# A shorter cosine chain, two heads' scores side by side, and an MLP output with columns on partitions

## The chip, the cores and the metric

The kernel runs on one core of a Trainium2 chip, in one launch. TensorE (PE) multiplies matrices and writes PSUM, VectorE (DVE), ScalarE (ACT) and GpSimd (POOL) work on SBUF and, but for GpSimd here, on PSUM, and SyncE (SP) issues the DMAs. The metric is the device time of the launch in microseconds. All engines run programs of their own in a fixed order and wait for each other by counters (semaphores).

## The reference

Attention over 4 batches, 8 heads, 576 positions and 64 columns, then two MLPs over 2304 tokens of 512 columns:

```python
def _attn_ref(q, k, v):
    factor = 4
    # mean over groups of 4 positions, full softmax attention on 144, repeated 4 times
    out_d = sm_attn(q_d, k_d, v_d)
    out_up = np.repeat(out_d, factor, axis=2)
    # plus attention in a band
    mask = np.abs(pos[:, None] - pos[None, :]) < factor
    scores = np.where(mask, scale * np.matmul(q, k.transpose(0, 1, 3, 2)), -1000000000.0)
    ...
    return out_up + out_local

def _moe_ref(x, w_in, w_out):          # d_ff 2048
    h = x @ w_in
    return (h * np.cos(h)) @ w_out

def _moe2_ref(x, w_gate, w_val, w_out, rms_g):   # d_ff 1536
    xn = x / np.sqrt(np.mean(x * x, axis=-1, keepdims=True) + 1e-06) * rms_g
    g = xn @ w_gate
    return (g / (1 + np.exp(-g)) * (xn @ w_val)) @ w_out
```

## The kernel before

**Stages.** Batch 0's attention comes first, with buffers of its own for every pair of heads (`Wide`). Then the first MLP runs over six chunks of 384 tokens; during chunks 0 to 2 the attention of batches 1 to 3 (`Narrow`, one set of buffers) is threaded between its steps. The second MLP runs over three chunks of 768 tokens, 12 units each, 36 iterations `i`, with the seven products of Strassen-Winograd type for gate and value (`product`) and the output tiles of the iteration before as fillers (`down2`). Each f32 operand of a large matmul is split into a high and a low part in `F32R`, and three matmuls (`three`) give one product.

**First MLP.** A unit `f` of 16 has a first layer, `up` (4 x 3 matmuls of 384 columns into a bank `HB`), and a second, `down`, three steps later. Before, `down` has the hidden values as stationary operand and writes three banks `YB` with tokens on partitions, nine matmuls of 512 columns. Between them, `cosines` (ScalarE) and `hidden` (VectorE) make g = h cos h: ScalarE adds a magic constant to h / 2 pi (L751), VectorE takes turns off (L1053, L1055), ScalarE takes the absolute value and the sine (L757, L759), VectorE multiplies (L1061), ScalarE writes the high part (L686) and VectorE the low (L972). The first layer of unit f may write its bank once the product of unit f-3 has read it (`g_done`).

**Attention in a chunk.** A pair of heads goes through steps placed by hand at (unit, half): TensorE's scores of head 0 (`local` for the band in ten windows, `downsampled` for the 144 means), then of head 1, `transposes` of each head's probabilities, `values`. They share banks X and Z, so head 1's scores wait for head 0's to be read. VectorE subtracts maxima, sums up and adds both attentions into XY (L893), ScalarE takes exponentials (L617, L626), GpSimd sums values of four positions (`value_sums`, L495 and L500) and normalises (L507, L510).

**After a chunk.** `squares` on ScalarE sums y's squares by token, GpSimd makes the reciprocal root (L549) and scales y (`scale_y`, L553). Because y has tokens on partitions and the second MLP needs columns there, TensorE turns the scaled y (`turn`, four transposes each, L1348): six turns in chunk 5, twelve in the second MLP, and VectorE copies them out with the gain (`turn_out`, L1006). From these come seven operands, each split in two parts (`operand_high`, `operand_low`).

**Weights of the second MLP.** During chunks 3 to 5 ScalarE, GpSimd and DMAs split 84 weight operands (`weight_high`, L722; `gate_sum`; `weight_low`, L578), two a unit, through three buffers `wp`, and store them.

Of the kernel before, what the change touches and what calls it, by code (L numbers as in the profile page):

```python
# [7 lines left out]
BF16 = mybir.dt.bfloat16  # L8
ACT = mybir.ActivationFunctionType
# [5 lines left out]
P = 128  # L15
# [4 lines left out]
DM = H * D  # L20
# [23 lines left out]
NWP = NP * F2  # L44
QT = SD // 2
# [36 lines left out]
def attention_and_two_mlps(nc, qk, vwin, vgrp, w1, wgv, w2, rms_g, const, wsplit, out):  # L82
# [41 lines left out]
    ssq = keep("ssq", [P, TT], F32)  # L124
    msq = keep("msq", [P, TT], F32)
    rinv = keep("rinv", [P, TT], F32)
    mhalf = keep("mhalf", [P, TT], F32)
    ones = keep("ones", [P, 1], F32)
    spare = keep("spare", [P, 4], F32)
# [27 lines left out]
    xa = at("xa", [P, KT, CH], F32, slots_at)  # L157
    xb = at("xb", [P, KT, CH], F32, slots_at + KT * CH * 4)
    xt = at("xt", [P, 3, 2, CH], F32, slots_at + 2 * KT * CH * 4)
    xo = at("xo", [P, NP, 2, 2, CH], F32R, slots_at + 5 * 4096 + 1024)  # L160
# [3 lines left out]
    wp = [at(f"wp{i}", [P, 2, 256], F32R, a) for i, a in enumerate((prep_at + 11264, prep_at + 13312, yn_at))]  # L164
# [15 lines left out]
    X, Z = ps[:, 3, :], ps[:, 7, :]  # L180

    NH = 3
    HB = [ps[:, i, 0:CH] for i in range(NH)]
    YB = [ps[:, 4 + i, :] for i in range(TT)]

    CA, CB = ps[:, 1, 0:CH], ps[:, 2, 0:CH]
    Y2 = [ps[:, i, :] for i in (3, 7, 0, 4, 5, 6)]

    def turn_bank(c, t):
        return ps[:, 2, :] if c else ps[:, (3, 7)[t % 2], :]  # L190
# [14 lines left out]
    class Narrow:  # L205
# [4 lines left out]
        sl, sd = [X[:, 0:TP * WIN]] * 2, [Z[0:QT, 0:2 * SD]] * 2  # L210
# [39 lines left out]
    turns_ready = sem("turns_ready")  # L250
    angle0 = sem("angle0")
    angle_ready = sem("angle_ready")
    abs_ready = sem("abs_ready")
# [6 lines left out]
    ssq_ready = sem("ssq_ready")  # L260
    ms_ready = sem("ms_ready")
    rinv_ready = sem("rinv_ready")
    y_scaled = sem("y_scaled")
    tr_done = sem("tr_done")
    turned = sem("turned")
# [9 lines left out]
    wp_stored = [sem(f"wp_stored{i}") for i in range(3)]  # L275
# [41 lines left out]
    def y_tile(c, t):  # L317
        return XY[:, bass.ds(c * (TT * 512) + t * 512, 512)]
# [4 lines left out]
    XSRC = [xa[:, 0:2, :], xa[:, 2:4, :], xt[:, 1], xt[:, 0], xb[:, 0:2, :], xt[:, 2], xb[:, 2:4, :]]  # L323
# [7 lines left out]
    POOL_XO = (1, 3, 5)  # L331
    XO_ORDER = ((0, 1, 3, 2, 4, 5, 6), (0, 1, 2, 3, 4, 5, 6))
    DVE_OUT, ACT_OUT = (0, 2, 4), (1, 3, 5)
    TURN_F = 1
    TURN_STEP = 5
# [26 lines left out]
    def steps_at(names, where, place):  # L362
        return [(name, j) for j in range(PAIRS) for name, at_ in zip(names, where[j]) if at_ == place]
# [6 lines left out]
    def sync_program(sp):  # L370
# [86 lines left out]
        for i in range(3):  # L457
            hold(sp, wp_stored[i], 16 * NWP // 3)
# [1050 lines left out]
```

## Time and profile before

| what | value |
|---|---|
| median of 3 runs | 992.53 us (990.57 to 994.08) |
| profiled execution, its own time | 996.6 us |
| its span in the trace | 994.5 us |
| TensorE busy | 960.3 us (97%) |
| VectorE, ScalarE, GpSimd busy | 575.5, 502.1, 313.2 us |
| mean granted clock of TensorE | 0.99 |

The span is the stretch from the first to the last instruction of one execution; its own time has the launch around it. Busy is the time in which an engine has an instruction in flight; matmuls overlap, so their durations add up to more than that, and the distance of their starts is their price. Most matmuls on f32 data appear as two records each. PEclk is the clock granted to TensorE as a share of full speed.

### The profile page before, as it was taken

The numbers are of one execution on the slowest core, as the hardware profiler recorded it, in microseconds if no ns is written. First come the engines' busy times: TensorE is split into PE (matmuls) and PEld (weight loads), VectorE is DVE, ScalarE is ACT, GpSimd is POOL, SyncE is SP. The second block draws the span as 40 slices with busy tenths as digits, with TensorE's granted clock in tenths as the row PEclk, the third lists the DMA queues.
The fourth block names the chain that finished last, engine by engine and source line by source line (L and its number), as shares of the span: only waits on it lengthen the run. The fifth ranks groups of instructions, "written<-read, shape, count | busy, mean of one in ns | idle before, by whom it ended". The sixth has DMA issues, their size and how long they took to land.

```text
span 994.5 us, 17685 instructions
## 1 busy us (share of the span) xinstructions
PE 960.3 (97%) x6104; PEld 853.5 (86%) x6104; DVE 575.5 (58%) x1225; ACT 502.1 (50%) x1081; POOL 313.2 (31%) x366
## 2 busy tenths in 40 slices
PE   7889999999999999999999899999999999999998
PEld 6677787888888899899989789999899899999997
DVE  6767677676666665555656644445744445544434
ACT  4456566666666667676765433334522224433322
POOL 5947773221322147467575121111300001000000
PEclk9999999999999999999999899999999999999999
DMA  9522111211111025445344575555565555575531
GB/s 306 192 94 93 55 52 36 70 52 53 52 53 53 23 100 177 149 159 180 132 166 149 190 258 153 151 150 162 151 215 150 150 166 160 156 226 158 161 106 64
DMA packets 66174, 132.31 MB, mean 133 GB/s; under 512 B 7088, under 2 KB 7216, under 8 KB 66096
## 3 DMA queue, kind: packets, MB, share of 16 engines
q1 hardware_dynamic: 66096, 131.27, 42.0%
q8 instruction: 50, 0.82, 0.3%
q14 instruction: 28, 0.23, 0.1%
HBM read 104.50 MB, written 26.74 MB: 132 GB/s over the span
## 4 chain that ended last, share of the span: by engine, by line
PE 78%; DVE 8%; ACT 6%; issue 4%; POOL 4%; DMA 1%; DVEq 0%; ACTq 0%; POOLq 0%; SPq 0%
PE ps L1274 24%; PE ps L1276 24%; PE ps L1275 24%; DVE ub L1053 2%; POOL W L521 2%; PE ps L1193 2%; DVE ub L1055 1%; ACT ub L757 1%; PE ps L1210 1%; ACT ub L759 1%; PE ps L1348 1%; DVE XY L893 1%; PE ps L1227 1%; ACT probd L626 1%; DVE ub L1061 1%
## 5 line engine op out<-in xcount | busy, mean ns | idle before, releaser
L1274 PE MATMUL ps<-xo,wu 128*128 128x384 f32 x504 | 169.7, 337 | 5.2 <-ACT gate_a L806 3.7
L1275 PE MATMUL ps<-xo,wu 128*128 128x384 f32 x504 | 170.7, 339 | 0.0
L1276 PE MATMUL ps<-xo,wu 128*128 128x384 f32 x504 | 170.1, 338 | 0.0
L1274 PE MATMUL ps<-xs,W 128*128 128x384 f32 x384 | 134.6, 350 | 1.4 <-DVE xs L968 1.4
L1276 PE MATMUL ps<-xs,W 128*128 128x384 f32 x384 | 130.8, 341 | 0.0
L1275 PE MATMUL ps<-xs,W 128*128 128x384 f32 x384 | 130.3, 339 | 0.0
L1274 PE MATMUL ps<-W,ring 128*128 128x512 f32 x288 | 118.0, 410 | 0.0
L1276 PE MATMUL ps<-W,ring 128*128 128x512 f32 x288 | 115.0, 399 | 0.0
L1275 PE MATMUL ps<-W,ring 128*128 128x512 f32 x288 | 114.8, 399 | 0.0
L1274 PEld LDWEIGHTS ps<-xo,wu 128*128 128x128 f32 x504 | 95.4, 189 | 12.4 <-ACT gate_a L806 4.1
L1275 PEld LDWEIGHTS ps<-xo,wu 128*128 128x128 f32 x504 | 95.2, 189 | 6.7
L1061 DVE TENSOR_TENSOR ub<-ub,ps 128x384 f32<-128x384 f32 x96 | 53.0, 552 | 74.0 <-ACT ub L759 74.0
L1276 PEld LDWEIGHTS ps<-xo,wu 128*128 128x128 f32 x504 | 95.3, 189 | 0.0
L757 ACT ACTIVATE ub<-ub 128x384 f32<-128x384 f32 x96 | 50.4, 525 | 72.5 <-DVE ub L1055 72.5
L1276 PE MATMUL ps<-wo,ring 128*128 128x512 f32 x216 | 85.7, 397 | 0.0
L1275 PE MATMUL ps<-wo,ring 128*128 128x512 f32 x216 | 85.4, 395 | 0.0
L1274 PE MATMUL ps<-wo,ring 128*128 128x512 f32 x216 | 85.2, 395 | 0.1
L1274 PEld LDWEIGHTS ps<-xs,W 128*128 128x128 f32 x384 | 73.2, 191 | 6.8 <-DVE xs L968 1.9
L1101 DVE TENSOR_TENSOR val_b<-val_b,ps 128x384 f32<-128x384 f32 x36 | 20.0, 554 | 101.1 <-ACT val_b L806 100.9
L1275 PEld LDWEIGHTS ps<-xs,W 128*128 128x128 f32 x384 | 73.3, 191 | 1.9
L1053 DVE TENSOR_SCALAR ub<-ub 128x384 f32<-128x384 f32 x96 | 47.3, 493 | 47.5 <-ACT ub L751 47.5
L1276 PEld LDWEIGHTS ps<-xs,W 128*128 128x128 f32 x384 | 73.1, 190 | 0.0
(134 smaller groups left out, 1853.3 us busy)
## 6 DMA issues: line engine op xcount, KB each, us to landing
wu<-wsplit SPq DMA_DIRECT2D x252, 256.0 KB, 2.8
wsplit<-wp SPq DMA_DIRECT2D x84, 256.0 KB, 2.0
W_raw<-w SPq DMA_DIRECT2D x8, 1024.0 KB, 14.1
qk<-qk SPq DMA_DIRECT2D x14, 576.0 KB, 4.1
gv<-wgv SPq DMA_DIRECT2D x12, 512.0 KB, 3.6
vw<-vwin SPq DMA_DIRECT2D x14, 384.0 KB, 3.2
out<-XY SPq DMA_DIRECT2D x18, 256.0 KB, 3.4
vg<-vgrp SPq DMA_DIRECT2D x26, 144.0 KB
```

Of the source, the lines that this page charges most:

```text
L521: g.tensor_tensor(lo, raw, hi.bitcast(F32), ALU.subtract).then_inc(unit_ready, 1)
L626: ins = a.activation(kind.probd[j][0:QT, s, t, :], kind.sd[s][:, t * SD:t * SD + SD], ACT.Exp, scale=SCALE_D, bias=dbias[0:QT, s, t:t + 1] ...
L757: a.activation(v, v, ACT.Abs).then_inc(abs_ready, 1)
L759: a.activation(v, v, ACT.Sin, scale=-1.0, bias=consts[:, 1:2]).then_inc(cos_ready, 1)
L893: ins = v.tensor_tensor(XY[:, bass.ds(first, m)].rearrange("p (n r) -> p n r", r=FACTOR), kind.pv[r][:, src:src + m].rearrange("p (n r) -> ...
L1053: v.tensor_scalar(w, w, MAGIC, -2.0 * math.pi, ALU.subtract, ALU.mult).then_inc(angle0, 1)
L1061: v.tensor_tensor(w, w, HB[f % NH], ALU.mult).then_inc(g_done, 1)
L1101: v.tensor_tensor(vb[:, :], vb[:, :], CB, ALU.add).then_inc(vb_ready, 1)
L1193: ins = t_.matmul(sl[64 * half:64 * half + 64, t * WIN:t * WIN + WIN], q[:, Q0[w]:Q0[w] + WIN], k[:, K0[w]:K0[w] + WIN], start=False, stop ...
L1274: t_.matmul(dst, a_lo, b_hi, start=first, stop=False, skip_group_check=True)
L1275: t_.matmul(dst, a_hi, b_lo, start=False, stop=False, skip_group_check=True)
L1276: return t_.matmul(dst, a_hi, b_hi, start=False, stop=last, skip_group_check=True)
```

## The change

1. The cosine: VectorE alone forms the turns from PSUM (h / 2 pi arrives scaled, since x is scaled where it is split), and ScalarE keeps the sine and the high part. `HB` has two banks, and the first layer of unit f waits for the product of unit f-2. The first layer of the next chunk's unit 0 moves ahead of this chunk's last second layer.
2. Scores of both heads stand side by side, head 0's in bank X, head 1's in bank Z, window by window. The steps of a pair are placed anew, with one pattern for all pairs.
3. `down` has the weights as stationary operand and writes y with columns on partitions into four banks, twelve matmuls of 384 columns. There are no turns.
4. Squares: GpSimd multiplies and adds up y's four parts, splits the sum (nine steps, `squares`), TensorE sums over partitions with a matrix of ones (`stats`), VectorE makes the reciprocal root from a bit trick and three Newton steps and scales y with the gain (`rms_step`).
5. Six `wp` buffers in place of three, nine operand slots in place of seven; operands of the second MLP's first chunk are made from step 5 of chunk 5 on, all low parts on VectorE.

```diff
-    NH = 3
+    NH = 2
     HB = [ps[:, i, 0:CH] for i in range(NH)]
-    YB = [ps[:, 4 + i, :] for i in range(TT)]
+    YB = [ps[:, 2 + k, 0:CH] for k in range(KT)]
+    STATS = X[:, 0:CH]
...
+        def squares(c, steps=range(2 * KT + 1)):
+            for n in steps:
+                k, adds = (n + 1) // 2, n and n % 2 == 0
...
+                elif adds:
+                    g.tensor_tensor(sq[:, 0, :], sq[:, 0, :], sq[:, 1, :], ALU.add).then_inc(sq_ready, 1)
...
+                    g.tensor_tensor(sq[:, min(k, 1), :], y_part(c, k), y_part(c, k), ALU.mult).then_inc(sq_ready, 1)
...
         batch(1, (5, 5, 5, 1))
         with pool.Fori(2, B) as b:
+            squares(b - 2)
             batch(b)
+        squares(ACH - 1)
...
+                for c, first in ((ACH, NP * 4), (ACH + 1, NP * 9)):
+                    if 0 <= NP * f + p - first <= 2 * KT:
+                        squares(c, (NP * f + p - first,))
...
-                a.activation(v, HB[f % NH], ACT.Identity, scale=INV_2PI, bias=consts[:, 0:1]).then_inc(turns_ready, 1)
...
-                a.activation(v, v, ACT.Abs).then_inc(abs_ready, 1)
-                act.wait_ge(abs_ready, F1 * c + f + 1)
-                a.activation(v, v, ACT.Sin, scale=-1.0, bias=consts[:, 1:2]).then_inc(cos_ready, 1)
+                a.activation(v, v, ACT.Sin, scale=-2.0 * math.pi, bias=consts[:, 1:2]).then_inc(cos_ready, 1)
...
-                v.tensor_scalar(w, w, MAGIC, -2.0 * math.pi, ALU.subtract, ALU.mult).then_inc(angle0, 1)
+                v.tensor_scalar(w, HB[f % NH], 0.25, MAGIC, ALU.add, ALU.add).then_inc(angle0, 1)
...
+                if before and not last and STAT + attention < f <= STAT + RMS_STEPS:
+                    rms_step(c - 1, f - STAT - 1)
...
-            return three(YB[t], ring[:, f % 3, 0, cols], ring[:, f % 3, 1, cols], w_part(slot, 0), w_part(slot, 1), f == 0, f == F1 - 1)
+            return three(YB[k], w_part(slot, 0)[:, cols], w_part(slot, 1)[:, cols], ring[:, f % 3, 0, :], ring[:, f % 3, 1, :], f == 0, f == F1 - 1)
...
+                if c and attention and step == 3:
+                    pe.wait_ge(exp_down, 2 * PAIRS * (c + 1) + 2)
+                    stats(c - 1, STATS)
+                elif c and not attention and not last and step == STAT:
+                    stats(c - 1, STATS)
```

The order of instructions shows three places. The first is TensorE in chunk 0, between the first layers of units 1 and 2, where the first pair's scores stand. Before (L1187 to L1190 are the masks, L1193 the ten windows of head 0, L1210 its downsampled scores):

```order
L1187 MATMUL ps<-maskb,identb 128x64 [waits qk_in,x_ready]
L1188 MATMUL ps<-maskb,identb 128x192
L1190 MATMUL ps<-maskb,identb 128x64
L1193 MATMUL ps<-qk_77 64x64 x10
L1210 MATMUL ps<-qkd_83 72x144 [waits qkd_ready]
L1210 MATMUL ps<-qkd_83 72x144
L1274 MATMUL ps<-xs,W_49 128x384 [waits g_done,unit_ready]
```

Now (L1192 to L1195 are the masks, L1201 the windows):

```order
L1192 MATMUL ps<-maskb,identb 128x64 [waits qk_in,x_ready]
L1193 MATMUL ps<-maskb,identb 128x192
L1195 MATMUL ps<-maskb,identb 128x64
L1192 MATMUL ps<-maskb,identb 128x64
L1193 MATMUL ps<-maskb,identb 128x192
L1195 MATMUL ps<-maskb,identb 128x64
L1201 MATMUL ps<-qk_80 64x64 x20
L1310 MATMUL ps<-xs,W_49 128x384 [waits g_done,unit_ready]
```

The windows of both heads come in one run, and the downsampled scores have moved behind the next first layer.

The second place is GpSimd's loop over batches 2 and 3, at the head of its body. Before, the loop begins at once with the value sums of the first pair:

```order
L557 UNCONDITIONAL_BRANCH
L557 ISA
L495 TENSOR_TENSOR vg_79<-vg_79 72x2x128 [waits vg_in]
L342 ISA
L500 TENSOR_TENSOR vd_80<-vg_79 72x2x64 [waits vt_ready,pv_done]
```

Now the last part of the squares (L567 adds a part, L561 and L564 split the sum) stands ahead of the value sums (L504, L509):

```order
L574 ISA [waits sq_ready,y_copied_act]
L574 TENSOR_TENSOR sq<-XY 128x384
L361 REGISTER_ALU
L567 TENSOR_TENSOR sq<-sq 128x384 [waits sq_ready]
L361 REGISTER_ALU
L561 TENSOR_TENSOR sums_of_sq<-sq,ones 128x384 [waits sq_ready,stat_done]
L361 REGISTER_ALU
L564 TENSOR_TENSOR sums_of_sq<-sq,sums_of_sq 128x384 [waits sshi_ready]
L361 ISA [waits sslo_ready]
L504 TENSOR_TENSOR vg_82<-vg_82 72x2x128 [waits vg_in]
L361 ISA
L509 TENSOR_TENSOR vd_83<-vg_82 72x2x64 [waits vt_ready,pv_done]
```

Nine steps of squares, of which these are the last four, have moved ahead of the first pair.

The third place is VectorE in chunks 1 and 2 at units 9 and 10, where the third pair's scores are handled. Now (L1068 and L1070 are the first two passes of the cosine, L883 the downsampling of q and k, L917 to L919 the downsampled maximum, L1009 to L1013 a Newton step):

```order
L883 TENSOR_REDUCE qkd_86<-qk_80 128x288 [waits down_scores,qk_in]
L1008 REGISTER_ALU
L1009 TENSOR_TENSOR sq<-rms 128x384 [waits newton]
L1010 REGISTER_ALU
L1011 TENSOR_TENSOR sq<-sq 128x384 [waits newton]
L1012 REGISTER_ALU
L1013 SCALAR_TENSOR_TENSOR rms<-sq,rms 128x384 [waits newton]
L1065 REGISTER_ALU
L1068 TENSOR_SCALAR ub<-ps 128x384 [waits glo_ready,up_done]
L1070 SCALAR_TENSOR_TENSOR ub<-ub,ps 128x384 [waits angle0]
L917 TENSOR_REDUCE dmax<-ps 72x2 [waits down_scores]
L919 TENSOR_SCALAR dbias<-dmax 72x2 [waits dmax_ready]
```

Before, the downsampling of the next pair stood at the previous pair's last step, ahead of the sums into XY (L893):

```order
L1055 TENSOR_TENSOR ub<-ub,ps 128x384 [waits angle0]
L943 COPY probd_82<-ps 72x288 [waits pt_done]
L880 REGISTER_ALU
L884 TENSOR_REDUCE qkd_83<-qk_77 128x288 [waits down_scores,qk_in]
L972 TENSOR_TENSOR ring<-ub,ring 128x384 [waits ghi_ready]
L1061 TENSOR_TENSOR ub<-ub,ps 128x384 [waits cos_ready]
L889 REGISTER_ALU
L893 ISA [waits od_ready]
L893 TENSOR_TENSOR XY<-ps,od_84 128x116
```

The downsampling has moved behind both heads' differences, and a Newton step of three passes follows it, ahead of the next unit's cosine.

## Rows read from the trace of the kernel before

**Rows 1.** The page's section 1: busy us, share of the span, instructions of each engine.

```profile
PE 960.3 (97%) x6104; PEld 853.5 (86%) x6104; DVE 575.5 (58%) x1225; ACT 502.1 (50%) x1081; POOL 313.2 (31%) x366
```

**Rows 2.** Windows of chunks 0, 1 and 4: length, busy of each engine, clock, DMA.

```profile
55.00:157.00 102.00, 97.19 (x797) 81.58 (x798) 71.83 (x182) 61.36 (x132) 61.95 (x65) 0.97 0.22 72
157.00:254.00 97.00, 94.10 (x803) 79.49 (x802) 66.29 (x176) 62.62 (x136) 25.68 (x37) 1.00 0.17 54
417.80:484.60 66.80, 66.80 (x337) 60.63 (x337) 38.18 (x71) 46.73 (x107) 45.48 (x56) 1.00 0.45 161
```

**Rows 3.** Timeline of TensorE in chunk 3: start, duration, line, tiles; first matmul of each layer.

```profile
401.26 0.39 PE L1274 MATMUL ps<-W,ring 128*128 128x512 f32 x1
...
403.34 0.33 PE L1274 MATMUL ps<-xs,W 128*128 128x384 f32 x1
...
405.45 0.39 PE L1274 MATMUL ps<-W,ring 128*128 128x512 f32 x1
```

**Rows 4.** The same in chunk 0: one head's scores, and the values of both.

```profile
61.73 0.20 PE L1187 MATMUL ps<-maskb,identb 128*128 128x64 bf16 x1
...
62.71 0.71 PE L1210 MATMUL ps<-qkd 64*72 64x144 f32 x4
...
63.35 0.44 PE L1274 MATMUL ps<-xs,W 128*128 128x384 f32 x1
...
80.27 0.71 PE L1243 MATMUL ps<-probd,vd 72*64 72x144 f32 x8
80.91 0.91 PE L1251 MATMUL ps<-prob,vw 64*64 64x58 f32 x40
81.75 0.50 PE L1274 MATMUL ps<-W,ring 128*128 128x512 f32 x1
```

**Rows 5.** Timeline: turns in chunk 5 and the second MLP, and L1096 without turns.

```profile
503.42 0.60 PE L1348 MATMUL ps<-ident,XY 128*128 128x128 f32 x4
503.78 0.42 PE L1274 MATMUL ps<-xs,W 128*128 128x384 f32 x1
...
583.27 0.63 PE L1348 MATMUL ps<-ident,XY 128*128 128x128 f32 x4
...
595.53 0.63 PE L1348 MATMUL ps<-ident,XY 128*128 128x128 f32 x4
...
861.46 0.55 DVE L1096 TENSOR_TENSOR gate_a<-gate_a,ps 128x384 f32<-128x384 f32 x1 [0.57 <-PE ps L1276]
...
872.97 0.56 DVE L1096 TENSOR_TENSOR gate_a<-gate_a,ps 128x384 f32<-128x384 f32 x1 [1.18 <-PE ps L1276]
```

**Rows 6.** Waits of TensorE: total, times, longest, us.

```profile
PE ps L1274 <- ACT gate_a L806: 3.7, 1, 3.7
...
PE ps L1187 <- DVE XY L893: 3.7, 5, 1.4
...
PE ps L1210 <- ACT probd L626: 3.6, 3, 1.7
...
PE ps L1348 <- DVE xa L1006: 2.2, 1, 2.2
```

**Rows 7.** Timeline of GpSimd at the start of chunk 1: value sums, normalising.

```profile
164.53 0.73 POOL L495 TENSOR_TENSOR vg<-vg 72x256 f32<-72x256 f32 x1
...
169.69 0.45 POOL L500 TENSOR_TENSOR vd<-vg 72x128 f32<-72x128 f32 x1 [0.18 <-POOL vg L495]
...
172.27 0.72 POOL L507 TENSOR_TENSOR prob<-prob,recip 128x320 f32<-128x320 f32 x1 [2.13 <-DVE recip L938]
173.18 0.67 POOL L510 TENSOR_TENSOR probd<-probd,recip 72x288 f32<-72x288 f32 x1 [0.18 <-POOL prob L507]
```

**Rows 8.** Groups by line and form: count | busy us, mean ns | idle before.

```profile
L578 POOL TENSOR_TENSOR wp<-gv,wp 128x256 fp32r<-128x256 f32 x48 | 38.9, 811 | 32.6 <-ACT wp L722 29.8
...
L884 DVE TENSOR_REDUCE qkd<-qk 128x288 f32<-128x1152 f32 x14 | 18.8, 1346 | 2.2 <-DMA qk<-qk 2.2
...
L1055 DVE TENSOR_TENSOR ub<-ub,ps 128x384 f32<-128x384 f32 x96 | 53.2, 554 | 3.3
```

More of the change, by code:

```diff
@@ L456, in sync_program @@
                 load_gv(f + 2)
-        for i in range(3):
-            hold(sp, wp_stored[i], 16 * NWP // 3)
+        for i in range(WPN):
+            hold(sp, wp_stored[i], 16 * NWP // WPN)
         for n in range(RING):
@@ L631, in exps @@
         def exps(kind, b, j, s):
-            if kind is Narrow and s == 0:
+            if kind is Narrow:
                 exp_of_down(kind, b, j, s)
@@ L688, in attend @@
         def attend(c, f, half):
-            for what, j in steps_at(BESIDE_STEPS, BESIDE_WHERE, (f, half)):
+            for what, j in steps_at(ACT_STEPS, ACT_AT, (f, half)):
                 if what == "exps":
@@ L1199, in downsampled, with downsampled_tile, scores @@
+        def downsampled_tile(kind, j, s, t):
+            q, k = (kind.qkd[j][64 * s:64 * s + 64, a, :] for a in range(2))
+            return t_.matmul(kind.sd[s][:, t * SD:t * SD + SD], q[:, t * QT:t * QT + QT], k, start=True, stop=True)
+        def scores(kind, b, j, s):
             n = PAIRS * b + j
             u = 2 * n + s
+            if u > 1:
+                pe.wait_ge(diff_ready, u - 1)
+            if s == 0:
+                pe.wait_ge(kind.qk_in[j], 16 * loads(kind, b, j))
+            masks(kind.sl[s])
+            for w in range(NW):
+                ins = local_window(kind, j, s, w)
+            ins.then_inc(local_scores, 1)
@@ L1201, in downsampled @@
             if s == 0:
                 pe.wait_ge(qkd_ready, n + 1)
[L1203 to L1206 removed]
+            if u > 1:
                 pe.wait_ge(exp_down, u - 1)
[L1208 removed]
             for t in range(2):
[L1210 removed]
+                ins = downsampled_tile(kind, j, s, t)
@@ L1211, in downsampled, with local_both @@
             ins.then_inc(down_scores, 1)
-        def scores(kind, b, j, s):
-            local(kind, b, j, s)
-            downsampled(kind, b, j, s)
+        def local_both(kind, b, j):
+            n = PAIRS * b + j
+            pe.wait_ge(x_ready, n)
+            pe.wait_ge(kind.qk_in[j], 16 * loads(kind, b, j))
+            for s in range(2):
+                masks(kind.sl[s])
+            for w in range(NW):
+                for s in range(2):
+                    ins = local_window(kind, j, s, w)
+            ins.then_inc(local_scores, 2)
@@ L1217, in transposes, with downsampled_both @@
+        def downsampled_both(kind, b, j):
+            n = PAIRS * b + j
+            pe.wait_ge(qkd_ready, n + 1)
+            pe.wait_ge(diff_ready, 2 * n + 2)
+            for t in range(2):
+                for s in range(2):
+                    ins = downsampled_tile(kind, j, s, t)
+            ins.then_inc(down_scores, 2)
         def transposes(kind, b, j, s):
             n = PAIRS * b + j
+            if kind is Narrow and j == 0 and s == 0 and b > 1:
+                pe.wait_ge(ms_ready, b - 1)
```

506 lines of the change are left out of this document (246 added, 260 removed), and 6 rows, old and new, of tables (BESIDE_WHERE, PE_WHERE).

## The prediction

> **What bounds it now.** I read the busy shares first: TensorE is busy for 960.3 of 994.5 us [rows 1]. The windows by chunk show where it isn't: 4.8 us idle in chunk 0 and 2.9 in chunk 1, which carry attention of the next batch, and none in chunk 4, which doesn't [rows 2]. VectorE is busy for 66 to 72 us of an attention chunk of about 100, ScalarE for 61 to 63, GpSimd for 62 in chunk 0 and 26 in chunk 1. So TensorE's own work sets the time, and a change gains what it takes off that stream and loses every wait that it puts in. The timeline gives the price of that work, the waits what is to be had: the table of waits holds single waits of 3.7 and 2.2 us around the second MLP's begin, 3.7 for attention's sums and 3.6 for the exponentials [rows 6].
>
> **The cosine chain.** It takes two of ScalarE's passes from each of 96 units and leaves VectorE three of them plus the low part, as before, 0.55 us each [rows 8]. In chunk 4 TensorE doesn't wait for this chain at all [rows 2], so the shorter chain itself is worth nothing. Its cover is the distance of two or three units between a unit's first layer and its second; with two PSUM banks for h in place of three, unit f+2 now waits for the product of unit f, which has a second layer and a first layer (4.2 us) to be made: three passes of 0.55, a sine and a low part of about the same are 2.8. If that cover went, each late unit would cost its lateness.
>
> **Columns on partitions in the first MLP's y.** Nine matmuls of 512 columns become twelve of 384. By [rows 3] nine take 403.34 - 401.26 = 2.08 us and twelve 405.45 - 403.34 = 2.11, so 96 units lose 0 to 3 us; I take 2.0.
>
> **No transposes.** The 18 turns go. The six in chunk 5 take 0.36 us each; the twelve in the second MLP make an iteration 12.26 instead of 11.51 us, 0.75 each [rows 5]: 2.2 + 9.0 = 11.2 us gained. Instead TensorE adds up squares: two matmuls of 384 columns for each of six chunks, 0.175 each [rows 3], 2.1 us, and 0.35 more for each of the two that wait for CB as the turns did: 2.8 us.
>
> **Both heads side by side.** One head's scores now take from 61.73 to 63.35, 1.62 us: 0.25 for the masks, 0.73 for ten windows, 0.64 for two downsampled tiles, and entries. Two heads take 3.3 per pair. The values step already alternates tiles of the array: 20 matmuls in 81.75 - 80.91 = 0.84 us, twice the rate of the windows, and four tiles of 144 columns in 80.91 - 80.27 = 0.64, twice the rate of the downsampled scores [rows 4]. If the new order reaches these rates a pair costs 0.5 + 0.84 + 0.64 = 2.0 to 2.1 and saves 1.24; 12 pairs save 14.9 us. The bounds are 0 and 14.9; I take the upper, since the new order alternates halves of both rows and columns. The Trainium skill (TensorE: Matmul & The Clock Gate, Part 3) has weights load beside a running matmul only when the row group differs, which would leave the old order without this overlap and give it to the new one; the trace agrees in the two rates, but shows no pair of row groups alone.
>
> **Waits taken away.** More room (six wp buffers, nine operand slots, operands scaled two chunks ahead) moves the second MLP's operands early, so I drop the 3.7 and the 2.2 us [rows 6]: 5.9 us gained. Of attention's 3.7 for the sums I drop 2.5: the addition no longer stands behind the downsampling of q and k.
>
> **Waits put in.** Here most of the gain goes.
> (a) GpSimd, start of chunks 1 and 2. Its program now does nine steps of 384 columns for the squares before anything of the next batch. 256 columns take 0.81 us [rows 8], so 384 take 0.81 to 1.22, I take 1.08 with the gap: 9.7 us, from 0.9 us after the last second layer (one product and one copy). Behind them the first pair's value sums take 170.14 - 164.53 = 5.6 us, a DMA in their middle, and the first head's normalising 1.6 [rows 7]: the first transposes can't start before 0.9 + 9.7 + 5.6 + 1.6 = 17.8 us. TensorE's own work up to there is three first layers (6.3), the scores (2.1), the sum (0.35) and one second layer (2.1): 10.9. It idles for 6.8 us in each of the two chunks, 13.6 us. Before, GpSimd had these sums done long before the first pair's transposes, and rescaled y in 3 x 1.1 us.
> (b) Chunk 0 has no squares. But reduction of q and k (1.35 us [rows 8]) now stands behind two heads' differences, a low part and a product, and the exponentials one step later; in the first two steps there is no second layer that hides it. TensorE waited 1.2 us a time there [rows 6]; with 1.35 more it waits some 2.3 for the downsampled scores and 2.1 for the transposes: 4.4 us. From (a) and (b), 18.0 us, the old 3.6 goes off.
> (c) In the last pair of each attention chunk both heads' transposes follow each other with no first layer between (unit 16 doesn't exist). The second needs both copies of the first, which stand behind a product: the product's 0.55 [rows 8], a copy that is no longer than that, and the hand-over, some 1.3 us, three times: 4.0.
> (d) VectorE's Newton steps, three dependent passes of 0.59 with the gap (1.8 us), stand behind steps 8, 9 and 10 of chunks 1 and 2, the middle pair's scores. VectorE has 97 - 66.3 = 31 us free per chunk [rows 2], but in these steps it is what the transposes wait for. Between 0 and 5.3 us per chunk; I take 3: 6.0.
> (e) Chunk 4: the squares are dealt out between the weights, one after each of nine. Nine weight steps and five gate sums at 0.82, and nine squares at 1.08, from 1.9 us after the chunk's begin: 1.9 + 11.5 + 9.7 = 23.1. TensorE asks for the sums at step 6, after six first layers and three second ones: 9 x 2.1 = 18.9. It waits 4.2 us (0 to 5).
> (f) The clock stood at half in part of chunk 0 (0.97 of full speed) and not in chunk 4 [rows 2]. It fell where TensorE had waited; some of these places go, others come. I put 0, with 5 us either way.
>
> **Sum.** -14.9 - 11.2 + 2.8 + 2.0 - 5.9 - 2.5 + 18.0 - 3.6 + 4.0 + 6.0 + 4.2 = -1.1 us on the profiled execution, whose span was 994.5 and own time 996.6. The runs' median is 992.5, so I forecast 991: 35 us of gain and nearly as much of new waiting. 3 us, 0.3%, is about what a measurement of this kernel tells from no change.
>
> **Rivals.**
> First, the new waits mostly don't come: (a) shrinks if GpSimd's squares or value sums are faster than their nearest rows, and (c) to (e) are of the kind that a queue some steps deep swallows. For it speaks that the old trace has few waits of TensorE at all [rows 6], though both other engines hand over at every step. Against it, the 17.8 us of (a) are four rows in one engine's fixed order. With (c) to (e) at zero and (a) halved: -1.1 - 14.2 - 6.8 = -22, 970 us. 0.27.
> Second, slower: the two heads' small matmuls don't overlap more than one head's did, because windows of one head already alternate halves of the columns. Then the 14.9 is missing: 1006 us. It decides from a pair's cost of 2.4 us upward (then the sum is over +3). Against it stands the rate of the values step. 0.12.
> Third, slower: GpSimd and VectorE hold each other up. Nothing in the old steps put long runs of GpSimd beside VectorE's work in chunks 1 and 2 (26 us of 97 busy [rows 2]); these chunks now have nine more GpSimd steps in one run each, beside the product chain. If each of the 18 costs 0.5 us on the way to the transposes, by one pass or another that has to be let by, that is +9: 1000 us. 0.15. The Trainium skill (SBUF — State Buffer, "Who interferes with whom") has a VectorE instruction with two SBUF inputs and a GpSimd one that reads SBUF exclude each other for the whole instruction; by it the first step of the cosine, which now reads PSUM, is free of this, and the Newton steps are not. No row shown here settles it.
> My own forecast, the new waits about eating the gain, has 0.44 and the range 984 to 998; 0.02 stays for anything else.
>
> **Chances.** Faster by over 0.3%: the first rival, 0.27, and 0.14 of my own case. Within 0.3%: 0.20 of my own, 0.04 of the others. Slower: 0.10 of my own and 0.25 of the rest. The range for 8 in 10 takes the first rival's 970 and goes up to between the second and third: 970 to 1003.
>
> **What would show it.** L1201, the windows of both heads, in about 0.84 us for 40 records, and the downsampled scores in 0.64 for 8. No wait at the second MLP's begin. At the start of chunks 1 and 2 nine squares in one run on GpSimd, and TensorE's first transposes waiting for its normalised probabilities, 17.8 us after the last second layer; a wait for the sums of 4 us at step 6 of chunk 4. The forecast is wrong if attention chunks are not longer idle than before, or if a pair's scores cost as much as they did.

## The result: 0.5% slower, by new waits larger than forecast and a lower clock

The changed kernel took a median of 997.49 us (995.44 to 1001.25) beside 992.59 us (990.55 to 996.51) for the kernel before on the same chip, 11 runs each. The ratio is 1.0054, with a 95% interval from 1.0037 to 1.0071. I had forecast 991 us, 0.1% faster: the measured time lies inside my range, but on the other side of no change. One execution of the run with short Newton steps below (1212.5 us at a mean granted clock of 0.716, the others at 989 to 994) was in a slow state and is left out.

The page of the changed kernel, its busy times:

```profile
PE 940.9 (94%) x6332; PEld 877.9 (88%) x6332; DVE 632.9 (63%) x1300; ACT 398.5 (40%) x863; POOL 338.0 (34%) x385
```

TensorE is busy for 19.4 us less than before [rows 1], and the span is 3.7 us longer (998.2): the change did take work off the engine that sets the time, and put in more waiting than it took: its idle time, span less busy, rises from 34.2 to 57.3 us, by 23.1. The windows of the changed kernel say where; the rows are chunks 0, 1, 2 and 4, then a stretch in chunk 1 (length, busy of PE, PEld, DVE, ACT, POOL, clock, DMA):

```profile
54.60:149.70 95.10, 86.80 (x838) 80.01 (x837) 69.02 (x180) 45.76 (x101) 60.94 (x65) 1.00 0.24 77
149.70:258.10 108.40, 94.59 (x851) 86.53 (x851) 75.53 (x191) 43.91 (x100) 30.47 (x41) 0.94 0.15 49
258.10:365.00 106.90, 93.66 (x852) 85.82 (x851) 75.93 (x191) 44.11 (x101) 30.30 (x41) 0.95 0.13 42
433.00:506.90 73.90, 70.20 (x388) 69.59 (x387) 54.51 (x87) 30.71 (x71) 49.41 (x60) 0.95 0.41 147
...
172.50:179.30 6.80, 5.05 (x19) 4.99 (x20) 0.45 (x1) 0.90 (x2) 3.49 (x5) 0.50 0.11 32
```

Against [rows 2], TensorE is idle for 13.8 us of chunk 1 in place of 2.9, for 3.7 of chunk 4 in place of none, and the clock of these chunks is 0.94 and 0.95 in place of 1.00. Chunk 0 is shorter, chunks 1 and 2 are 10 to 12 us longer. The table of TensorE's waits (what it waited for, total, times, longest), to be set beside [rows 6]:

```profile
PE ps L1263 <- POOL probd L519: 16.5, 13, 1.7
PE ps L1207 <- DVE qkd L883: 10.5, 8, 2.6
PE ps L1263 <- issue: 8.5, 2, 4.5
...
PE ps L1336 <- POOL sums_of_sq L564: 3.0, 1, 3.0
...
PE ps L1310 <- DVE ub L1078: 1.8, 3, 0.7
```

L1263 are the transposes, L1207 the downsampled scores, L1336 the sum of squares, L1310 a first layer. The 3.7 us at the second MLP's begin and the 2.2 for xa are gone, as forecast. All of the waits shown are in the first MLP's chunks.

The first gain is to be seen in TensorE's timeline of chunk 0, changed kernel (start, duration):

```profile
61.43 0.20 PE L1192 MATMUL ps<-maskb,identb 128*128 128x64 bf16 x1
...
61.81 0.81 PE L1201 MATMUL ps<-qk 64*64 64x64 f32 x40
62.55 0.44 PE L1310 MATMUL ps<-xs,W 128*128 128x384 f32 x1
...
67.10 0.71 PE L1207 MATMUL ps<-qkd 64*72 64x144 f32 x8 [2.17 <-DVE qkd L883]
67.74 0.44 PE L1310 MATMUL ps<-xs,W 128*128 128x384 f32 x1
```

Both heads' masks and windows take 62.55 - 61.43 = 1.12 us and both heads' downsampled scores 0.64. A pair costs 1.76 in place of 2 x 0.98 + 2 x 0.64 = 3.24 [rows 4]: 1.5 us less, 18 over 12 pairs.

The largest loss is at the start of chunk 1. GpSimd there, changed kernel:

```profile
155.47 0.83 POOL L574 TENSOR_TENSOR sq<-XY 128x384 f32 x1 [9.68 <-DVE XY L1057]
...
164.84 1.17 POOL L564 TENSOR_TENSOR sums_of_sq<-sq,sums_of_sq 128x384 fp32r<-128x384 f32 x1 [0.18 <-POOL sums_of_sq L561]
166.40 0.72 POOL L504 TENSOR_TENSOR vg<-vg 72x256 f32<-72x256 f32 x1 [0.38 <-POOL sums_of_sq L564]
...
170.70 0.99 POOL L504 TENSOR_TENSOR vg<-vg 72x256 f32<-72x256 f32 x1 [2.84 <-DMA vg<-vgrp]
...
172.59 0.72 POOL L516 TENSOR_TENSOR prob<-prob,recip 128x320 f32<-128x320 f32 x1 [0.27 <-POOL vd L509]
173.49 0.66 POOL L519 TENSOR_TENSOR probd<-probd,recip 72x288 f32<-72x288 f32 x1 [0.18 <-POOL prob L516]
```

Nine passes from 155.47 to 166.01, the first head's value sums, a DMA for the second head's that GpSimd waits 2.84 us for (it is issued only when the single buffer is free), and the normalising to 174.15. TensorE's transposes at that place and of the third pair of the same chunk:

```profile
174.25 0.87 PE L1263 MATMUL ps<-ident,prob 128*128 128x128 f32 x3 [4.48 <-issue]
...
223.12 0.55 PE L1263 MATMUL ps<-ident,prob 128*128 128x128 f32 x3 [1.72 <-POOL probd L519]
...
227.73 0.55 PE L1263 MATMUL ps<-ident,prob 128*128 128x128 f32 x3 [1.68 <-POOL probd L519]
```

The first starts at 174.25, 0.1 us after the end of GpSimd's pass over probd: the profile names no releaser ("issue"), but this is it, as the first experiment bears out. It is 20.3 us behind the last second layer of chunk 0, where I had 17.8. The third pair waits for VectorE. Its timeline ahead of the transposes at 227.73:

```profile
221.00 0.54 DVE L1009 TENSOR_TENSOR sq<-rms 128x384 f32<-128x384 f32 x1
221.58 0.96 DVE L1011 TENSOR_TENSOR sq<-sq 128x384 f32<-128x384 f32 x1
222.57 0.90 DVE L1013 SCALAR_TENSOR_TENSOR rms<-sq,rms 128x384 f32<-128x384 f32 x1
223.40 0.54 DVE L1068 TENSOR_SCALAR ub<-ps 128x384 f32<-128x384 f32 x1
...
224.45 0.48 DVE L930 TENSOR_REDUCE sums<-prob 128x5 f32<-128x320 f32 x1
...
225.17 0.20 DVE L937 RECIPROCAL recip<-sums 128x7 f32<-128x7 f32 x1
```

A Newton step, two passes of the cosine, and only then the sum over head 1's exponentials, from which GpSimd takes another 2.3 us to the transposes.

### The profile page after: what moved, and what is told of

Read it like the earlier page. It is cut to its first block, busy times and chain, and to the rows that moved or that the text cites. A ratio compares the mean times of both kernels' runs of the same rounds, so it can differ in the third digit from the quotient of the medians.

```text
span 998.2 us, 17970 instructions
## 1 busy us (share of the span) xinstructions
PE 940.9 (94%) x6332; PEld 877.9 (88%) x6332; DVE 632.9 (63%) x1300; ACT 398.5 (40%) x863; POOL 338.0 (34%) x385
## 4 chain that ended last, share of the span: by engine, by line
PE 75%; DVE 9%; POOL 6%; issue 5%; ACT 3%; DMA 1%; DVEq 0%; SPq 0%; POOLq 0%; ACTq 0%
PE ps L1310 24%; PE ps L1312 23%; PE ps L1311 23%; POOL W L530 2%; DVE qkd L883 1%; DVE ub L1068 1%; ACT L647 1%; PE ps L1263 1%; PE ps L1287 1%; POOL prob L516 1%; POOL probd L519 1%; DVE ring L971 1%; DVE ub L1070 1%; PE ps L1279 1%; ACT probd L647 1%
## 5 line engine op out<-in xcount | busy, mean ns | idle before, releaser
L1310 PE MATMUL ps<-xo,wu 128*128 128x384 f32 x504 | 168.6, 335 | 1.5 <-DVE gate_a L1110 1.5
L1310 PE MATMUL ps<-xs,W 128*128 128x384 f32 x384 | 134.9, 351 | 3.2 <-DVE ub L1078 1.8
L1310 PE MATMUL ps<-ring,W 128*128 128x384 f32 x384 | 133.7, 348 | 0.0
L1312 PE MATMUL ps<-ring,W 128*128 128x384 f32 x384 | 130.6, 340 | 0.0
L1311 PE MATMUL ps<-ring,W 128*128 128x384 f32 x384 | 130.3, 339 | 0.0
L772 ACT ACTIVATE ub<-ub,consts 128x384 f32<-128x384 f32 x96 | 59.2, 617 | 154.4 <-DVE ub L1070 153.4
L1310 PEld LDWEIGHTS ps<-xo,wu 128*128 128x128 f32 x504 | 94.7, 188 | 8.1 <-DVE gate_a L1110 1.8
L1068 DVE TENSOR_SCALAR ub<-ps 128x384 f32<-128x384 f32 x96 | 53.0, 553 | 53.6 <-PE ps L1312 53.4
L1310 PE MATMUL ps<-wo,ring 128*128 128x512 f32 x216 | 84.3, 390 | 0.1
L1310 PEld LDWEIGHTS ps<-xs,W 128*128 128x128 f32 x384 | 74.3, 194 | 7.0 <-issue 4.1
L1310 PEld LDWEIGHTS ps<-ring,W 128*128 128x128 f32 x384 | 73.5, 191 | 2.5 <-issue 1.7
L1311 PEld LDWEIGHTS ps<-xs,W 128*128 128x128 f32 x384 | 74.5, 194 | 0.0
L1312 PEld LDWEIGHTS ps<-xs,W 128*128 128x128 f32 x384 | 74.2, 193 | 0.0
## 6 DMA issues: line engine op xcount, KB each, us to landing
W_raw<-w SPq DMA_DIRECT2D x8, 1024.0 KB, 13.8
```

The source lines that it names most:

```text
L772: a.activation(v, v, ACT.Sin, scale=-2.0 * math.pi, bias=consts[:, 1:2]).then_inc(cos_ready, 1)
L1068: v.tensor_scalar(w, HB[f % NH], 0.25, MAGIC, ALU.add, ALU.add).then_inc(angle0, 1)
L1310: t_.matmul(dst, a_lo, b_hi, start=first, stop=False, skip_group_check=True)
L1311: t_.matmul(dst, a_hi, b_lo, start=False, stop=False, skip_group_check=True)
L1312: return t_.matmul(dst, a_hi, b_hi, start=False, stop=last, skip_group_check=True)
```

## Experiments

The first six change one thing each on the changed kernel, the later ones stand on the run of four parts. Every run has 5 to 12 executions, with executions of the kernel before beside them. I compare ratios to the kernel before, since the chip's own time moved by up to 0.7 us between groups of runs; their intervals are some 0.0015 either way, so a difference below 0.002 (2 us) is not told from none. Where I compare executions at one clock, it is the mean granted clock that each of them has on record.

| run | median, us | ratio | 95% interval |
|---|---|---|---|
| changed kernel | 997.5 | 1.0054 | 1.0037 to 1.0071 |
| squares late | 984.6 | 0.9920 | 0.9904 to 0.9936 |
| heads one after the other | 1002.8 | 1.0105 | 1.0091 to 1.0118 |
| q and k early | 999.9 | 1.0076 | 1.0062 to 1.0089 |
| Newton short | 990.9 | 0.9986 | 0.9974 to 0.9999 |
| sums later | 994.2 | 1.0022 | 1.0010 to 1.0034 |
| last pair split | 994.5 | 1.0022 | 1.0011 to 1.0032 |
| four parts together | 976.8 | 0.9849 | 0.9829 to 0.9868 |
| and Newton spread | 976.0 | 0.9838 | 0.9822 to 0.9854 |
| four parts, local exponentials first | 972.6 | 0.9796 | 0.9782 to 0.9810 |
| four parts, two Newton steps | 971.1 | 0.9775 | 0.9757 to 0.9793 |
| four parts, both of these | 966.4 | 0.9740 | 0.9726 to 0.9754 |
| the same, q and k late | 967.6 | 0.9757 | 0.9743 to 0.9770 |

### Squares behind the first pair

```diff
+                if j == 0 and squares_of is not None:
+                    squares(squares_of)
...
-            squares(b - 2)
-            batch(b)
+            batch(b, squares_of=b - 2)
...
-            if kind is Narrow and j == 0 and s == 0 and b > 1:
+            if kind is Narrow and j == 1 and s == 0 and b > 1:
...
-                if c and attention and step == 3:
+                if c and attention and step == 7:
...
-                if before and attention and f == 3:
+                if before and attention and f == 7:
```

> GpSimd's squares of chunks 0 and 1 stand behind the first pair's value sums and normalising, and TensorE's sum of them, VectorE's reading of it and the wait of the transposes move from unit 3 to unit 7. Theory A (the fixed order squares, value sums, normalising holds the first pair's transposes): the two waits of 4.5 and 4.1 us at 174 and 282 us go, with them the half clock that follows, and nothing is late instead: 8 to 12 us less than the changed kernel's 997, about 987. Theory B (GpSimd's length, not its order, is what costs): the second pair's transposes wait instead, or the sum of squares does, and the time stays within 2 us.

13.3 us less (1.0054 to 0.9920): theory A, and by more than it said. Waits of TensorE in this run, and its chunks 1 and 2:

```profile
PE ps L1264 <- POOL probd L519: 16.9, 14, 1.9
PE ps L1208 <- DVE qkd L884: 10.0, 10, 2.0
```

```profile
151.90:253.00 101.10, 90.61 (x852) 82.96 (x851) 74.92 (x191) 43.98 (x99) 30.21 (x41) 0.98 0.16 52
253.00:354.00 101.00, 92.11 (x851) 84.33 (x850) 75.01 (x191) 44.10 (x101) 29.09 (x39) 0.97 0.14 44
```

The two long waits are gone; at the same transposes 2.05 and 0.51 us stay. All waits of the two first pairs together (worked out as in the section on why) fall from 15.6 to 8.0 us. The two chunks are 13.2 us shorter: TensorE is idle for 7.7 us less and busy for 5.5 us less, with the same matmuls, and the clock is 0.98 and 0.97 in place of 0.94 and 0.95. So order on GpSimd, not its length, was the larger cost, and a part of it came through the clock.

### Heads one after the other

```diff
-            for w in range(NW):
-                for s in range(2):
+            for s in range(2):
+                for w in range(NW):
                     ins = local_window(kind, j, s, w)
```

and the same for the two downsampled tiles.

> Only the order within a step changes back: all ten windows of head 0, then all of head 1, and the same for the downsampled scores. Banks, steps and waits stay. Theory A (the alternation of heads is what made a pair cost 1.77 us in place of 3.3): the 20 windows take 2 x 0.73 again and the downsampled scores 2 x 0.64, 1 us or more per pair, 12 to 18 us in all: 1009 to 1015. Theory B (the separate banks and the missing entries between the heads did it, not the alternation): under 3 us more, below 1001.

5.1 us more. Neither theory holds (12 to 18 us, under 3 us): the alternation is worth 5 of 18 us. TensorE in chunk 0 of this run:

```profile
62.40 1.21 PE L1201 MATMUL ps<-qk 64*64 64x64 f32 x40
63.54 0.44 PE L1310 MATMUL ps<-xs,W 128*128 128x384 f32 x1
...
67.86 0.72 PE L1207 MATMUL ps<-qkd 64*72 64x144 f32 x8 [1.95 <-DVE qkd L883]
68.51 0.45 PE L1310 MATMUL ps<-xs,W 128*128 128x384 f32 x1
```

The windows take 1.14 us in place of 0.74, 0.4 a pair, which is the 5 us. The downsampled scores take 0.65 either way, no more than one head's alone before [rows 4]. So the larger part came from having both heads in one run, without a large matmul between: ten windows of one head alone took 0.73 us [rows 4], and ten more behind them add 0.41 here and nothing when the heads alternate. It needed separate banks for the heads, but no alternation.

### q and k downsampled one unit earlier

```diff
-    DVE_AT = ((0, 0), (0, 1), (1, 0), (1, 1), (2, 0), (2, 1), (3, 0), (3, 1))
+    DVE_AT = ((0, 0), (-1, 1), (1, 0), (1, 1), (2, 0), (2, 1), (3, 0), (3, 1))
```

> VectorE's downsampling of q and k goes one unit ahead, behind the previous pair's addition into XY and ahead of this pair's differences. Theory A (the downsampled scores wait because the reduction of 1.35 us stands behind two heads' differences, a low part and a product): the 10.5 us of waits for qkd at the downsampled scores go, and little comes: 8 to 12 us less than the changed kernel, about 988. Theory B (VectorE's queue is full there and any place costs the same): the wait moves to the second layers (low part of g) or the exponentials, and the time stays within 2 us.

2.2 us more (at the edge of what can be told), so theory A falls. Theory B comes near to the time, but not to the place where the wait went. In TensorE's waits of this run:

```profile
PE ps L1263 <- POOL probd L519: 16.5, 12, 2.6
PE ps L1336 <- POOL sums_of_sq L564: 8.5, 3, 3.0
...
PE ps L1207 <- DVE prob L911: 2.6, 5, 1.3
```

The 10.5 us for qkd are gone. 2.6 stay at the same place for the differences, and the sum of squares is waited for 5.5 us longer, since TensorE comes to it sooner and GpSimd doesn't.

### Newton steps short in the attention chunks

```diff
+                if not isinstance(c, int):
+                    x, y, r = x[:, 0:2], y[:, 0:2], r[:, 0:2]
```

> In the attention chunks the three Newton steps work on 2 of 384 columns (the reciprocal roots of chunks 0 and 1 are then left at the first guess), so that each pass keeps its place and its waits but hardly any length. Theory A (term (d): VectorE is what the third pair's transposes wait for in units 8 to 10): 4 to 6 us less than the changed kernel, 992. Theory B (VectorE has room enough for 1.8 us a unit): no difference, within 1.5 us.

6.7 us less: theory A, a little above its range. The wait for the normalised probabilities falls from 16.5 to 9.4 us:

```profile
PE ps L1265 <- POOL probd L519: 9.4, 12, 1.4
```

### Sums of chunks 3 and 4 one unit later

```diff
-                elif c and not attention and not last and step == STAT:
+                elif c and not attention and not last and step == STAT + 1:
```

and the same for VectorE's steps on the sum in these chunks.

> In chunks 3 and 4 TensorE's sum of squares and VectorE's eight steps on it come one unit later (7 in place of 6); attention chunks stay. Theory A (term (e): GpSimd's squares between the weights end 3 us after TensorE asks for them in chunk 4, and a unit is 4.2 us long): the wait of 3.2 us and the half clock behind it go, 3 to 6 us less than the changed kernel, 993. Theory B (the weights of GpSimd and ScalarE are what is short there, and the wait moves): within 1 us.

3.2 us less: theory A, at its lower end. Chunk 4 of this run:

```profile
434.60:502.50 67.90, 67.22 (x387) 66.73 (x386) 53.88 (x86) 30.71 (x71) 51.05 (x60) 1.00 0.44 159
```

It is 6.0 us shorter than in the changed kernel, for a wait of 3.2: the clock is 1.00 in place of 0.95, since the stretch at half behind the wait is gone too. The profiled execution as a whole is 4.3 us shorter: in its chunk 0 the clock is 0.98 in place of 1.00.

### The last second layer split

```diff
+                split = attention and step == F1
+                if split:
+                    second_layer(c, step - 3, (0, 1))
                 if attention:
                     attend(c + 1, step, 0)
...
+                if split:
+                    second_layer(c, step - 3, (2, 3))
```

> At unit 16 of an attention chunk two of the four parts of unit 13's second layer stand between the last pair's first and second transposes, the other two ahead of the values. Theory A (term (c): the second transposes wait for the copies of the first with nothing between): three waits of 1.3 us go, 3 to 5 us less than the changed kernel, 993. Theory B (the copies hang on VectorE's queue and come later still): within 1.5 us.

3.2 us less, theory A. The last pair's two transposes of chunk 1, where the second now has a filler and waits 0.21 us (1.31 in the changed kernel):

```profile
247.31 0.55 PE L1263 MATMUL ps<-ident,prob 128*128 128x128 f32 x3 [0.84 <-POOL probd L519]
...
249.42 0.55 PE L1263 MATMUL ps<-ident,prob 128*128 128x128 f32 x3 [0.21 <-POOL probd L519]
```

### Four parts together

Squares late, q and k early, sums later, last pair split.

> The squares behind the first pair, q and k downsampled one unit earlier, the sum of chunks 3 and 4 one unit later, and the last second layer split, together. Theory A (the early downsampling gained nothing by itself only because the squares of the same chunks took what it gave): with the squares out of the way it gains its 8 us, and the parts add up: 985 - 8 - 4 - 4 = 969. Theory B (VectorE's queue is full in attention chunks, so that the early downsampling costs what it gains with the squares late too): 985 - 8 + 0 to 3 = 977 to 980.

20.3 us less than the changed kernel (1.0054 to 0.9849), 1.5% faster than the kernel before. The three parts that gained alone add up to 19.7, so the early downsampling still brings nothing that can be told (0.6): theory B. Its waits:

```profile
PE ps L1264 <- POOL probd L519: 16.9, 14, 2.6
...
PE ps L1208 <- DVE prob L912: 2.3, 5, 1.3
```

### Newton steps in other units

```diff
+                if before and attention:
+                    for step in {8: (1,), 11: (2,), 12: (3,), 13: (4,), 14: (5,), 15: (6, 7)}.get(f, ()):
+                        rms_step(c - 1, step)
```

> The last but with the Newton steps of the attention chunks in units 8, 11 and 12 in place of 8, 9 and 10, and the scaling of y in 13, 14 and 15 (two parts in the last). Theory A (the Newton steps cost time in units 9 and 10, where the third pair's scores wait for VectorE, and a place after its sums hides them): 4 to 6 us less than the run before it, of the 6.6 that the short passes gained. Theory B (any place in these chunks costs the same 1.8 us a step): within 1.5 us of the run before it.

0.0011 less in ratio, no difference: theory B. The third pair's waits shrink (in chunk 1 from 2.72 and 0.44 us to 0.82) and the fourth's grow (from 0.79 to 1.82 and 1.83); the total for probd is 17.7 us beside 16.9.

### Local exponentials first

```diff
-                exp_of_down(kind, b, j, s)
                 exp_of_local(kind, b, j, s)
+                exp_of_down(kind, b, j, s)
```

> The run with all four parts (977 us), and ScalarE takes each head's local exponentials ahead of its downsampled ones, so that VectorE's sum over them runs beside ScalarE's next passes. Theory A (what is left of the waits is one chain per pair, from the downsampled scores by ScalarE, VectorE and GpSimd to the transposes, and every piece taken off it counts): head 0's chain is 0.3 to 0.5 us shorter, and the 14 waits for its normalised probabilities shrink by 3 to 5 us: 973. Theory B (VectorE's and ScalarE's queues are full, and order inside a step is worth nothing): within 1 us.

5.3 us less than the four parts alone. No work is left out; only the order inside one step of ScalarE changed. Theory B falls, and the time is what theory A said, but the waits bear it out only in part:

```profile
PE ps L1264 <- POOL probd L519: 15.1, 12, 2.1
```

The first wait of the first pair of chunk 1 is 2.05 us in place of 2.50, so the chain is 0.45 shorter, as expected. But the waits for probd fall by 1.8 us in all, not 3 to 5, others grow, and TensorE's idle time in the profiled executions is 37.2 us beside 37.6; it is its busy time that fell, by 3.6. The clock has its part in this: the median is 0.995 in place of 0.991. Executions at one clock differ by less than 5.3 us: 973.3 beside 975.9 at 0.993, 972.0 beside 975.7 at 0.996 (one of each).

### Two Newton steps

```diff
-NEWTON = 3
+NEWTON = 2
...
+                    for step in {8: (1,), 11: (2,), 12: (3,), 13: (4,), 14: (5,), 15: (6,)}.get(f, ()):
+                        rms_step(c - 1, step)
```

So the places change too, and the run with the steps spread is the nearer one to compare with.

> The run with all four parts, with two Newton steps in place of three everywhere (the reciprocal root is then good to about 5 millionths); in attention chunks they stand in units 8 and 11, the scaling in 12 to 15. Theory A (VectorE's load in attention chunks is what costs, wherever it stands): three passes of 0.59 less in each of two chunks, and no more than one step in a unit: 2 to 3 us less, 974. Theory B (only a step in units 9 and 10 costs): the same as the run with the steps spread, 976.

7.3 us less than the four parts and 6.3 less than the run with three steps spread, where theory A had 2 to 3. Theory B falls. The passes that went are 2 x 1.8 = 3.6 us in these chunks. The clock is higher too (median 0.995 beside 0.992); at one clock, 0.995, the spread run took 974.9 us and this one 971.1, 3.8 less (one execution each), which is about the passes that went.

### Both, and q and k late again

> Both of the last two together. If their gains are of one kind (one chain per pair) they add up: 970 to 972. If the second only fills what the first has freed, it stays at the better of the two, 973.

10.8 us less than the four parts; the parts were 5.3 and 7.3. Within the noise they add up, as the expectation has it for gains of one kind; the time lies under its 970 us because both parts had gained more than forecast. This is the fastest kernel, 2.6% under the one before. Its windows (chunks 1 and 2) and waits:

```profile
146.20:239.80 93.60, 88.89 (x851) 81.64 (x851) 72.78 (x188) 44.06 (x99) 30.63 (x41) 1.00 0.18 57
239.80:335.00 95.20, 90.46 (x852) 83.28 (x851) 72.81 (x188) 44.35 (x101) 30.41 (x39) 0.98 0.15 47
```

```profile
PE ps L1267 <- POOL probd L519: 11.5, 11, 2.0
```

TensorE idles 4.7 us in each of chunks 1 and 2, and the mean clock of the profiled execution is 0.998 in place of 0.985.

> The last run (966 us) with the downsampling of q and k put back to where the changed kernel has it, behind both heads' differences. Theory A (term (b): the place costs 0.8 us of a wait in every pair and more in the first of a chunk, and this shows once nothing else holds the same pair up): 6 to 10 us more, 972 to 976. Theory B (as in the changed kernel, the pair's chain ends at the same time wherever the reduction stands): within 2 us of 966.

```profile
PE ps L1211 <- DVE qkd L884: 10.3, 10, 2.2
PE ps L1267 <- POOL probd L519: 8.5, 9, 1.5
```

0.0017 more, theory B. With the reduction late TensorE waits 10.3 us for qkd and 8.5 for probd; with it early 11.5 for probd and 2.3 for the differences. The wait for qkd is real, but about half of it is waited anyway, one step on, and the rest shows in the time by 1.7 us at most.

## Why the prediction was wrong

The mechanism was right: TensorE's work falls by about 25 us, and waits, most of them in the attention chunks, eat it. What failed is the size of the waits put in: terms (a) to (e) had 32.2 us, and 43 came, with 4.2 of them where (b) had none and 2.3 at the two h banks, which I had put at nothing; and the clock, term (f), which I had put at zero. Together these changed the side of no change on which the time ends. Waits are taken here from the distances of starts in the timeline, less the work between, those above 0.4 us.

- **Heads.** -14.9 forecast. The own time of a pair fell by 1.5 us, 18. The size was off because the new pair costs 1.76 where I had 2.0 to 2.1: 0.38 for the masks in place of 0.50, 0.74 for the windows in place of 0.84. The reason was off too: the alternation gives 5 us, the common run the rest.
- **Turns, sums, 384 columns.** -11.2 + 2.8 + 2.0 forecast, together -6.4. The second MLP from its second iteration on is 7.7 us shorter, beside -7.6 for its share of these terms, and the six turns of chunk 5 are gone, 2.2. Chunk 3, its wait taken out, is 67.2 us beside 66.8: 0.43 a chunk, 2.6 for six, where I had 3.4. Together -7.3: these held to 1 us.
- **Waits taken away.** They went as forecast, and with them what I had left of those for the sums (4.5 us went, where I had 2.5) and 1.1 us at the transposes of the first pairs of chunks 0 and 1. In all 16 us where I had 5.9 + 2.5 + 3.6 = 12.
- **(a).** 13.6 forecast. The first pairs of chunks 1 and 2 wait 2.77 + 0.53 + 4.65 and 2.55 + 0.84 + 4.23: 15.6. The chain to the first transposes was 20.3 and 19.7 us, for 17.8: a GpSimd pass with its gap takes 1.17, not 1.08 (10.54 / 9), and the squares began 1.5 us after the last second layer, not 0.9. The value sums and the normalising took what I had, with the DMA in their middle. I had also counted no wait ahead of the sum, where 2.6 to 2.8 us for qkd stand; it adds nothing by itself, since GpSimd ends last.
- **(b).** 4.4 forecast for chunk 0's first pair; 2.34 + 1.84 came. Outside the first pair I had nothing, and a wait of 0.8 to 0.9 stands in five further pairs: 4.2. But the experiments give this place as such about 2 us at most (2.2 more, 0.6 less, 1.7 less with the reduction early): the same pair then waits longer at its transposes.
- **(c).** 4.0 forecast. The two transposes take 2.51 us in place of 1.10 in chunk 0 (2.72 in chunk 1, and 3.34 in chunk 2, partly at half clock); at 1.4 us each this is 4.2, and in chunks 1 and 2 the first of them waits 1.02 and 0.80 besides: 6.0. Splitting a second layer got 3.2 back.
- **(d).** 6.0 forecast; 1.89 + 1.85 in each of two chunks is 7.5, and the short steps gained 6.7.
- **(e).** 4.2 forecast, 3.2 came.
- **The two h banks** weren't free, where I had argued that a second and a first layer cover the chain: at the start of a chunk, where no second layer stands between, a first layer waits 0.66 to 0.85 us once in each of three chunks, 2.3.
- **(f), the clock.** Zero forecast, "5 us either way". In the profiled executions the mean granted clock fell from 0.99 to 0.985: 15.0 us of full speed missing from 998.2 beside 9.9 from 994.5, 5 us. Counted only while TensorE is busy, in windows of 1 us, it is 13.7 beside 9.9: 3.8. These two executions show less than the rest: the medians are 0.995 for the kernel before (58 executions beside the experiments) and 0.984 for the changed one (11), 11 us missing, and what a missing microsecond costs in the kernel before (last section) makes that an estimated 5 to 6 us, about the whole of the measured difference. It fell behind new waits: in chunk 1 it is 0.50 (1.2 of 2.4 GHz) from 172.5 to 179.3, where TensorE's wait of 4.5 us ends, and in the run without that wait the chunk has 0.98. Not behind all: after the 2.34 us at 67.10 it stays at 1.00. I had argued that some places go and others come; more came than went, and why one wait is followed by half clock and another isn't stays open.

New waits as found, without the clock: 15.6 + 4.2 + 4.2 + 6.0 + 7.5 + 3.2 + 2.3 = 43 us, less 16, is +27, where my sum had +20. With -18 - 7.3 = -25.3 of work this gives +1.7, no more than the sum leaves open: by it, without the clock the two kernels are about equal. With +3.8 of clock it is +5.5. The span rose by 3.7 (23.1 idle, less 19.4 busy). The 1.8 us between are open: half clock ahead of a wait may only shorten that wait, which would take off a part, but no run shows it by itself.

**The rivals.** The first (waits mostly don't come) is refuted by the table of waits. The second (heads don't overlap) is refuted by a pair's 1.76 us, well under the 2.4 from which it decides; even with the heads one after the other a pair costs 2.2. The third (GpSimd and VectorE hold each other up) ended nearest to the time, but its mechanism carries little of it. Passes of VectorE with two SBUF inputs did take about 1 us in place of 0.55 beside GpSimd, 0.96 and 0.90 in the rows above; that lengthens one Newton step of three in each chunk by 0.75 us. GpSimd's own passes beside VectorE's are longer too: the third pair's normalising took 0.86 and 0.76 us for head 0 and 0.83 and 1.12 for head 1, where the first pair's took 0.72 and 0.66. So at most some 1.5 us of the third pair's 3.7 in each of two chunks is of this kind. In chunks 3 and 4 a low part of g of 1.02 and 1.05 us stands ahead of the product that a first layer waits for (0.82 and 0.85 us); in chunk 5, where the low part took 0.55, that wait is 0.66.

**What was missing as a view.** I read VectorE's 31 us free in 97 as room. Each pair runs through one chain of three engines (scores, maxima, exponentials, sum, reciprocal, normalising, transposes), with the cosine's passes between its pieces. TensorE waits at its end, though each of the three has free time. So shortening the Newton steps, 10.8 us of VectorE in two chunks, gained 6.7, and other places for them gained nothing; the reduction mattered by 2 us at most wherever it stood; and 0.45 us off ScalarE's part of the chain gained 3 to 5 us over 12 pairs, a part of it by the clock.

## To carry to other kernels

Before an engine with free time gets work, find the chain that runs through it with a deadline, and count the distance of this chain's end from the instruction that waits; the busy share doesn't show it. Work that nobody needs soon belongs behind the first link that somebody waits for: moving the same nine GpSimd passes from ahead of the first pair to behind it gained 13 us. When a change removes work from TensorE and adds waits, put a term for the clock into the sum.

## What the runs showed of the hardware

The clock went with the waits. From the changed kernel over the four parts to the fastest kernel the mean granted clock of the profiled executions is 0.985, 0.988, 0.998, and the median of all executions 0.984, 0.991, 0.996, with times of 997, 977, 966 us. It also differs between executions of one kernel: of the kernel before, 11 at 0.991 have a median of 993.8 us and 34 at 0.995 one of 991.7, so that 4.0 us of full speed missing cost 2.1 us. At one clock the kernels still differ: at 0.996 the four parts took 975.7 us (one execution) and the fastest kernel 966.2 to 966.5 (three). So some 9 of the 10 us between these two don't need the clock.

VectorE's low part of g (L971, two SBUF inputs) and its first pass of the cosine (L1068, from PSUM), groups of the changed kernel (count, busy, mean ns):

```profile
L971 DVE TENSOR_TENSOR ring<-ub,ring 128x384 fp32r<-128x384 f32 x96 | 67.3, 701 | 10.3 <-ACT ring L707 10.1
...
L1068 DVE TENSOR_SCALAR ub<-ps 128x384 f32<-128x384 f32 x96 | 53.0, 553 | 53.6 <-PE ps L1312 53.4
```

Both handle 128x384; one takes 701 ns on average and the other keeps to 553. Single passes show it: in chunk 3, beside a GpSimd pass from 372.19 to 373.21, the low part is

```profile
372.60 1.02 DVE L971 TENSOR_TENSOR ring<-ub,ring 128x384 fp32r<-128x384 f32 x1
```

and the cosine's first pass, at 371.54 beside GpSimd's squares, took 0.56. The Trainium skill (SBUF — State Buffer, "Who interferes with whom") has only the first kind shut out by a GpSimd instruction that reads SBUF; the trace agrees.

A change of ScalarE's function cost its table load and nothing more. In the run of four parts, ScalarE between a sine and the exponentials:

```profile
160.98 0.62 ACT L773 ACTIVATE ub<-ub,consts 128x384 f32<-128x384 f32 x1 [0.53 <-DVE ub L1071]
161.61 1.28 ACT L648 ACT_TABLE_LOAD   x1
162.91 0.38 ACT L648 ACTIVATE probd<-ps,dbias 72x144 f32<-72x144 f32 x1
```

From the sine's end at 161.60 to the next pass at 162.91 are 1.31 us; of the 24 switches in the attention chunks of this run 22 take 1.30 to 1.32 us, and in the other two ScalarE waits for VectorE. The Trainium skill (ScalarE: Activation LUTs, "What ACT_TABLE_LOAD costs") gives 1283 ns for the load, as here, and 1380 ns of draining beside it, which don't show here. This load stands in every pair's chain, twelve times.
